# Attention units taken chunk by chunk through the batches, with two narrow first groups and stores by tile

## What is computed

```python
f = 1.0 / (1.0 + np.exp(-f_logit))
for t in range(S):
    state = f[:, :, t, :, None] * state + einsum('bhd,bhe->bhde', k[:, :, t], v[:, :, t])
    y[:, :, t] = einsum('bhd,bhde->bhe', q[:, :, t], state)
x = y as (B * S, H * D)                      # 3072 tokens of 384
h = x @ w_in                                 # 384 -> 2048
x = (maximum(h, 0) + log1p(exp(-abs(h)))) @ w_out
h = x @ moe2_w_in
x = where(h >= 1, h, where(h <= -1, 0, (h + 1)**2 / 4)) @ moe2_w_out
```

## Time and profile before

| | |
|---|---|
| median of three runs | 954.64 us (952.54 to 954.88) |
| profiled execution, its own time | 954.34 us |
| its span, first to last instruction | 952.6 us |
| TensorE matmuls busy | 909.5 us, 95% |
| VectorE, ScalarE, GpSimd busy | 538.1, 446.2 and 84.6 us |
| mean granted TensorE clock | 0.985 |
| bytes moved by DMA | 49.8 MB, mean 52 GB/s |

### The profile page before, as it was taken

One profiled execution on the slowest core, in us unless ns is written; L12 is line 12 of the kernel. 1 busy time (PEld: TensorE's weight loads), 2 busy tenths in 40 slices (PEclk: granted clock), 3 DMA queues, 4 the chain that ended last, 5 costly groups with the idle time before them and its releaser, 6 DMA issues.

```text
span 952.6 us, 14831 instructions
## 1 busy us (share of the span) xinstructions
PE 909.5 (95%) x5742; PEld 765.7 (80%) x5742; DVE 538.1 (56%) x925; ACT 446.2 (47%) x837; POOL 84.6 (9%) x66
## 2 busy tenths in 40 slices
PE   5569999899999999999999999999999999999996
PEld 3469999889778787877888888888888888888885
DVE  4965576665655656566435555455555554554543
ACT  3465666556554655565467743233323333332322
POOL 3321021211210111012000010000000000000000
PEclk8789999999999999999999999999999999999998
DMA  9631133223212132131012210020010200200001
GB/s 214 190 94 40 39 81 63 57 55 64 65 40 55 57 71 47 40 119 54 1 67 86 81 67 0 1 67 1 20 47 0 67 1 1 67 1 1 33 1 36
DMA packets 18811, 49.77 MB, mean 52 GB/s; under 512 B 1968, under 2 KB 3120, under 8 KB 18736
## 3 DMA queue, kind: packets, MB, share of 16 engines
q1 hardware_dynamic: 18736, 48.77, 19.5%
HBM read 39.32 MB, written 9.44 MB: 51 GB/s over the span
## 4 chain that ended last, share of the span: by engine, by line
PE 87%; DVE 6%; issue 3%; ACT 2%; DMA 2%; POOL 0%; SPq 0%; DVEq 0%; ACTq 0%; POOLq 0%
PE h_ps L464 13%; PE y_ps L464 13%; PE h_ps L466 13%; PE y_ps L466 13%; PE h_ps L465 13%; PE y_ps L465 13%; PE a_ps L521 2%; PE c_ps L534 2%; PE a_ps L554 2%; DVE dec L805 1%; DVE g_lo L786 1%; PE c_ps L541 1%; PE c_ps L547 1%; PE c_ps L511 1%; DMA w_raw<-w 1%
## 5 line engine op out<-in xcount | busy, mean ns | idle before, releaser
L786 DVE TENSOR_TENSOR g_lo<-gate,g_hi 128x512 fp32r<-128x512 f32 (+2 forms) x208 | 142.4, 685 | 337.8 <-ACT g_hi L648 337.8
L464 PE MATMUL h_ps<-x_hi,w_hi 128*128 128x512 f32 (+2 forms) x624 | 238.0, 381 | 8.9 <-DVE gate L770 7.2
L464 PE MATMUL y_ps<-g_hi,w_hi 128*128 128x512 f32 (+2 forms) x624 | 234.3, 376 | 9.0 <-DVE y_sb L792 4.7
L465 PE MATMUL h_ps<-x_lo,w_hi 128*128 128x512 f32 (+2 forms) x624 | 233.3, 374 | 0.0
L466 PE MATMUL h_ps<-x_hi,w_lo 128*128 128x512 f32 (+2 forms) x624 | 233.2, 374 | 0.0
L466 PE MATMUL y_ps<-g_hi,w_lo 128*128 128x512 f32 (+2 forms) x624 | 232.7, 373 | 0.0
L465 PE MATMUL y_ps<-g_lo,w_hi 128*128 128x512 f32 (+2 forms) x624 | 232.7, 373 | 0.0
L636 ACT ACTIVATE soft<-h_ps 128x512 f32<-128x512 f32 x96 | 57.4, 598 | 260.0 <-PE h_ps L466 260.0
L464 PEld LDWEIGHTS y_ps<-g_hi,w_hi 128*128 128x128 f32 x624 | 117.6, 188 | 32.5 <-DVE g_lo L786 13.7
L464 PEld LDWEIGHTS h_ps<-x_hi,w_hi 128*128 128x128 f32 x624 | 117.7, 189 | 31.6 <-DVE w_lo L867 7.7
L632 ACT ACTIVATE soft<-h_ps 128x512 f32<-128x512 f32 (+2 forms) x112 | 60.1, 536 | 166.5 <-PE h_ps L466 166.4
(11 more groups left out here) (76 smaller groups left out, 660.9 us busy)
## 6 DMA issues: line engine op xcount, KB each, us to landing
qkf_sb<-qkf SPq DMA_DIRECT2D x48, 288.0 KB, 5.0
w_raw<-w SPq DMA_DIRECT2D x32, 384.0 KB, 5.3
v_sb<-v SPq DMA_DIRECT2D x24, 320.0 KB, 5.3
qkf_sb<-x_mid SPq DMA_DIRECT2D x6, 768.0 KB, 6.2
out<-y_sb SPq DMA_DIRECT2D x6, 768.0 KB, 3.9
x_mid<-y_sb SPq DMA_DIRECT2D x4, 768.0 KB, 4.0
x_mid<-y_sb SPq DMA_DIRECT2D x2, 576.0 KB, 3.4
x_mid<-y_sb SPq DMA_DIRECT2D x1, 384.0 KB, 2.8
```

What stands on the lines that cost most here:

```text
L464: nc.tensor.matmul(out_ap, hi1, hi2, start=start, stop=False, skip_group_check=True)
L465: nc.tensor.matmul(out_ap, hi1, lo2, start=False, stop=False, skip_group_check=True)
L786: nc.vector.tensor_tensor(g_lo[:, t % 2, 0:g.n], gate[:, t % 2, 0:g.n], g_hi[:, t % 2, 0:g.n].bitcast(F32), ALU.subtract).then_inc(glo_don ...
```

## The change

- **Order of the units.** Unit u is now chunk u // 4 of batch u % 4. The state is kept for each batch; the first four units have no state to read and the last four leave none. The host lays the inputs out so, and turns the output back.
- **First groups.** Layer 0 has groups of 2, 2, 4, 4, 4, 4, 4 units instead of 3, 2, 3, 4, 4, 4, 4. The prologue does units 0 and 1 with their own buffers (scores and turned keys of unit 1 in y_sb), with keys and queries multiplied on VectorE and the plus one on ScalarE. Weight slices 0 to 2 get their low part from GpSimd, 3 from VectorE; slices 4 to 15 are split in group 0's slots (`first_splits`), four slots ahead of their use. The increments of units 0 and 1 stand behind `up(0)` and `up(1)`. Units 2 and 3 have their main stages spread over slots m to m + 4.
- **Loads.** The padding rows come from DRAM; the memsets are gone. A unit has three loads with semaphores of their own: f, qk and v (112 rows of 2 KB and of 4 KB, 128 rows of 2 KB).
- **State and v.** The state is 64 columns a pair, read by TensorE without stride: eight matmuls with 48 rows and four with 112. v has 64 columns a head. The increment is eight matmuls of 64 or 48 stationary columns by 64 instead of four of 112 by 96. VectorE updates the state with two operations of 112 rows instead of four of 48.
- **Slots.** MAIN for 4 units is (0, 4, 8, 12) instead of (2, 5, 9, 12). The last scan and the second Newton operation come behind g_lo in their slot (`prep_end`). `dec` has two buffers.
- **Tiles stored singly.** Each y_ps tile has its own semaphores, ScalarE copies tile 0 as soon as it is complete, and each tile is stored by its own DMA.

```diff
-SIZES = ((3, 2, 3, 4, 4, 4, 4), ...
-MAIN = {2: (4, 9), 3: (3, 7, 11), 4: (2, 5, 9, 12)}
+SIZES = ((2, 2, 4, 4, 4, 4, 4), ...
+MAIN = {2: (7, 12), 3: (3, 7, 11), 4: (0, 4, 8, 12)}
 PREP = (-5, -4, -3, -1)
-STAGES = 4
+STAGES = (0, 1, 2, 3)
+EARLY_STAGES = (0, 1, 3, 4)
+EARLY_STAGES_PE = (0, 2, 3, 4)
...
+        def first_splits(slot):
+            return range(slot + 4, min(slot + 5, FT)) if slot > 2 else range(EARLY, slot + 5)
...
+                load_f(0)
+                load_f(1)
+                load_qk(0)
+                load_qk(1)
+                load_v(0)
+                load_v(1)
+                for m in range(4):
+                    load_w(m)
+                load_unit(2)
+                for m in range(4, RAW):
+                    load_w(m)
+                for m in range(RAW, RAW + 3):
+                    load_w(m)
                 unit_left(0)
                 load_unit(3)
+                load_w(RAW + 3)
+                unit_left(1)
+                load_unit(4)
...
+                for k in range(KT):
+                    sp.wait_ge(y_ps_free[k], g.G + 2)
+                    sp.dma_start(to[:, k, g.token:g.token + g.n], y_sb[:, k, 0:g.n]).then_inc(y_sb_free, 16)
...
+            def increment(u):
+                a_ps, kt = banks(u)[0], k_tok_of(u)
+                for p in range(PAIRS):
+                    for a, cols in ((0, slice(0, 64)), (1, slice(64, ROWS))):
+                        h = 2 * p + a
+                        mm = nc.tensor.matmul(a_ps[cols, p * HEAD:(p + 1) * HEAD], kt[:, p, cols],
+                                              v_sb[:, u % RING, h * HEAD:(h + 1) * HEAD],
+                                              start=True, stop=True, skip_group_check=True)
...
+            pe.wait_ge(consts, 6)
             keep_warm(3)
-            first_group(prep, main, no_split)
-            keep_warm(1)
+            turn_keys(0)
+            keep_warm(2)
+            turn_keys(1)
+            keep_warm(3)
+            score(0)
+            score(1)
+            result(0)
+            result(1)
             up(LAYER0[0], 0)
             up(LAYER0[0], 1)
+            increment(0)
+            increment(1)
+            pe.wait_ge(state_done, FIRST)
...
             def copy_y(g):
-                act.wait_ge(y_done, FT * (g.G + 1))
-                act.wait_ge(y_sb_free, 16 * (g.G + 1))
-                for k in range(2):
-                    nc.scalar.activation(y_sb[:, k, 0:g.n], y_ps[k][:, 0:g.n], ACT.Copy).then_inc(y_ps_free, 1)
+                act.wait_ge(y_sb_free, 16 * KT * (g.G + 1))
+                for k in range(KT - 1):
+                    act.wait_ge(y_tile_done[k], g.G + 1)
+                    nc.scalar.activation(y_sb[:, k, 0:g.n], y_ps[k][:, 0:g.n], ACT.Copy).then_inc(y_ps_free[k], 1)
...
+            prep(0, 1)
+            prep_end(0, 1)
+            keys(0)
+            prep(1, 1)
+            prep_end(1, 1)
+            keys(1)
+            prep(0, 3)
+            prep_end(0, 3)
+            queries(0)
+            prep(1, 3)
+            prep_end(1, 3)
+            queries(1)
+            main(0, 1)
+            main(1, 1)
+            main(0, 3)
+            main(1, 3)
+            split_w(3)
             gated(LAYER0[0], 0)
+            main(0, 2)
             split_lo(LAYER0[0], 0)
-            rest_of_first(prep, split_w)
+            main(1, 2)
```

More of the change, by code:

```diff
@@ L102, in prep_at, with batch, has_past, has_future @@
         return []
[L103 to L111, removed]
+    return [(u, PREP.index(at - m)) for u, m in MAIN_SLOT.items() if at - m in PREP]
+def batch(u):
+    return u % B
+def has_past(u):
+    return u >= B
+def has_future(u):
+    return u < UNITS - B
+def states_until(u):
+    return min(u + 1, UNITS - B)
 def build(nc, qkf, v, w, out, x_mid):
@@ L539, in main @@
                         for j in range(4):
-                            h = 4 * tile + j
-                            nc.tensor.matmul(c_ps[HALF * j:HALF * (j + 1), t], v_sb[:, slot, h * D:h * D + HALF],
-                                             scores[:, h % 2, h // 2, :], start=False, stop=True, skip_group_check=True)
+                            pair, rows = 2 * tile + j // 2, slice(64 * (j % 2), 64 * (j % 2) + D)
+                            nc.tensor.matmul(c_ps[HALF * j:HALF * (j + 1), t], st[rows, pair, 0:HALF],
+                                             q[rows, pair, :], start=(tile == 0), stop=False, skip_group_check=True)
@@ new lines, in result @@
+                pe.wait_ge(v_in[u % RING], 16 * (u // RING + 1))
+                pe.wait_ge(masked, 2 * u + 2)
+                for tile in range(2):
+                    t = slice(tile * P, (tile + 1) * P)
+                    for j in range(4):
+                        h = 4 * tile + j
+                        nc.tensor.matmul(c_ps[HALF * j:HALF * (j + 1), t], v_sb[:, u % RING, h * HEAD:h * HEAD + HALF],
+                                         sc[:, h % 2, h // 2, :], start=(tile == 0 and not has_past(u)),
+                                         stop=True, skip_group_check=True)
@@ L564, in body, with main @@
+            def main(u, s):
+                if s == 0:
+                    turn_keys(u)
+                    score(u)
+                if s == 1:
+                    result(u)
+                    if has_future(u):
+                        increment(u)
             def body(g):
@@ L893, in body @@
                     gated(of, t)
+                    for m in first_splits(slot) if g.G == 0 else ():
+                        split_w(m)
                     for u, s in main_at(g, slot):
```

438 lines of the change are left out of this document (208 added, 230 removed).

## The result

The changed kernel takes 920.58 us (median of four runs, 918.61 to 925.53) against 953.72 for the kernel before on the same chip: a ratio of 0.966, 95% interval 0.962 to 0.970. The forecast was 936.5, with a range of 925 to 949. The sign is right, the gain of 33 us is nearly twice the 18 forecast, and the time lies outside the range.

A forecast was written before the change was run, and what follows sets the result against it. The prediction took TensorE to bound the kernel: its wait before the first feed-forward matmul, its work and its standing. Its terms summed to -18.0 us from 954.34, giving 936.3 in the profiled execution, stated as 936.5, range 925 to 949.

The forecast's parts named there:

- First `up`: Prologue: the first feed-forward matmul starts at about 21.5 us instead of 45.46, -24.0 us.
- One more unit, increments of units 0 and 1, no state for 2 and 3: TensorE work behind the first `up`: +4.0 us, +1.6 us and -1.4 us.
- New shapes: Increment and state blocks: smaller tiles, taken to overlap in pairs, cost +1.5 us, range -1 to +12.
- Group 0: First group's body: 15 us of TensorE standing instead of 9.5, three engines equally full, +5.5 us.
- feeds keep up: ScalarE and VectorE run ahead, group 0 loses 9 us, not 15, and boundary waits vanish: 929 us; chance 0.24.
- The two-unit group: Group 1: four units prepared beside 256-wide slots instead of three, +1.5 us.
- Wide groups: 4-wide boundaries and slots: 8.9 us of layer 0 waits fall to 3.5 us, -5 us, bounds -8 and +2.
- Tail: End of the run: the last tile, stored singly, is issued earlier and lands sooner, -1.7 us.
- Unpaired increments: Increment block: column tiles do not overlap in pairs, +8 us; 944.5 us, chance 0.23 shared with a starved group 0.
- Starved group 0: Group 0: weight slices 9 and up queue behind unit loads, +7 us; 944.5 us, chance 0.23 shared with unpaired increments.
- Half clock in the narrow groups: Two narrow groups: the granted clock stays at half, 965 us with 20 slow slots; chance 0.04.
- Late prologue: Prologue: unit loads hold the first matmul to 40 us or later, giving 955 us; chance 0.02.

The follow-up runs named there:

- f4: Changed kernel without the eight useless `keep_warm` matmuls in the prologue; 923.39 us.
- f3: Changed kernel with nine extra, unused ScalarE copies of 512 columns ahead of weight splits in group 0; 922.41 us.
- e3: Changed kernel with the last scan and second Newton operation ahead of the weight split (g_lo) on VectorE again; 921.36 us.
- f1: Changed kernel with slots 2, 5, 9, 12, last scan and second Newton step ahead of g_lo, whole copies and one store; 925.64 us.
- f5: Changed kernel with slots 2, 5, 9, 12 and each unit's preparation whole ahead of g_lo, unit by unit; 932.87 us.
- g1: Kernel before with `dec` twice and preparations split, second parts after all first parts, still ahead of g_lo; 945.59 us against 952.75.
- g2: Kernel before with only the main parts of 4-unit groups moved to slots 0, 4, 8, 12; 943.01 us, ratio 0.989.
- e4: Changed kernel with one store and one wait for the three y_ps tiles instead of single ones; 921.76 us.
- f2: Changed kernel with old slots, old order ahead of g_lo, one store, and the state update in four operations of 48 rows; 927.79 us.
- i1: Changed kernel with the wait for the first two states put behind `up(2)` and unit 3's main stage one slot earlier; 922.61 us.

## Why the prediction was wrong

**First `up`: -24.0 forecast, -25.5 measured.** The chain of the text gave 19.7, and 19.95 came; f landed at 3.9, the scans start at 5.32 as forecast, the qk load was late by 0.9 us. The failed step is the addition of 1.8 us for `keep_warm` and loads. f4 shows that the extra matmuls shorten the chain. That 19.7 fits within 0.3 us is in part luck, as the late load was not in it.

**One more unit, increments of units 0 and 1, no state for 2 and 3: +4.2 forecast.** By the counts of blocks in both traces this is +4.3.

**New shapes: +1.5 forecast, -1.4 measured** (20 increments, each 0.2 us less, and 20 state blocks, each 0.13 more). I took pairs to overlap but no gain from it, though the figure used, 16 instructions at 29 ns, already gave 0.46 against the 0.81 of the old block. The upper figure of +4 took the 0.1 us of one change for each of the drains that the Trainium skill ("TensorEngine Tiling (Array Packing)", Key Properties) tells of at a change of tiling mode. It fell: the state block with its 48-row tiles and its change of mode costs 0.13 us more in all. With +0.3 us for slots of 256 instead of 384 columns these terms give the +3.1 of the account within 0.1 us.

**Group 0: +5.5 forecast, -1.4 measured.** Before, it stood 11.2 us, not 9.5. After, it stood 9.8, not the 15 of the forecast, and here the failed step is "if each slot took what its longest engine takes the group would be 57". The rows of the windows view (length, busy time of PE, PEld, DVE, ACT, POOL, granted clock, DMA share, GB/s) for group 0 from slot 2 to slot 2, and for most of the two-unit group:

```profile
24.46:77.77 53.31, 47.43 (x516) 43.96 (x516) 43.88 (x85) 40.52 (x96) 9.00 (x7) 1.00 0.39 123
77.77:126.00 48.23, 47.83 (x569) 44.62 (x566) 36.00 (x79) 30.85 (x78) 9.07 (x7) 1.00 0.30 89
```

ScalarE has 40.5 us of work where I had put 45, VectorE 43.9 for 41, and the group takes 53.3, with 4.0 us for the two blocks of unit 4 in it that the 57 leaves out. The engines run ahead of each other between waits, so an uneven slot is made good by the next; f3 shows it directly, 5.4 us more work for 2.2 us more time, clock included. The order of the preparation has little share: undone alone it cost 2.2 us in this group, 1.5 of them by the clock (e3), undone with the slots nothing (f1, f5). The rival "feeds keep up" named this and gave 929, for which it lacked the next points.

**The two-unit group: +1.5 forecast, -0.6 measured.** The step took four units beside narrow slots to overfill ScalarE and VectorE. It holds for the old order and slots: in f5 this group takes 62.2 us, nearly half of the excess by the clock, in the changed kernel 54.2. The forecast gave the new order no credit here.

**Wide groups: -5 forecast, -10.3 measured.** The step that failed is the cause given for the earlier trace rows and the 3.5 us of waits that it left standing: "a copy of y_sb stands behind preparation on VectorE". That is so, but the preparation was 1 us longer than its work, and I had priced slots by the usual duration of their instructions. All 8.9 us of the eight gaps went. Had I listed the durations of the scans along the run, eight of them at 2.35 would have stood out. g1, g2 and f5 show this cause: standing in the wide groups changes by -6.9, -10.1 and +5.1 us, the whole times by -7.2, -9.7 and +12.3. The meeting itself is 0.98 us of VectorE a time, 8 us in sum; what stays open is how the rest divides. g2 takes away the slow scans and also spreads other work, and f5 still stands less in the wide groups than the kernel before (11.0 against 16.2 us, in groups that are not the same). No run has f5's edits and the single store together.

**Tail: -1.7 forecast, +0.5 measured.** The median landing did fall, to 2.2 us on the page. But in this execution the last store took 5.2 us to land, 1.4 of them its issue: three issues in a row take 3.07 us on the queue, which the forecast, with one issue at 0.38, left out. By all profiles (see e4) the term is about -1, and the +0.5 belongs to this pair of executions.

**Rivals.** Unpaired increments: refuted by 0.61 us. Starved group 0: refuted by its 9.8 us. Half clock in the narrow groups: refuted, granted clock 1.00 in both windows above; but spells of 3.4 or 6.8 us at 0.50 came there in e3, f2, f3, f4, f5 and i1, so its mechanism exists, only far shorter than the rival had it. Late prologue: refuted by 19.95.

## What to carry to other kernels

List the duration of one instruction along the run, not only its mean: where the same shape takes 1.37 us in one slot and 2.35 in another, see which other engine runs beside it. An order that keeps VectorE's two-input work away from GpSimd's products where a slot has no time left can be worth 1% without an instruction less, and it shows in an undo experiment only when everything that keeps them apart is undone together. Before a term of 1 or 2 us is judged by one pair of profiles, look at the same term in the others. A sum of each slot's longest engine overstates the time of a group whose engines may run ahead.

## What the runs showed of the hardware

- Four scans on VectorE of 1.37 us take 2.35 beside a GpSimd product, g_lo 1.24 instead of 0.69, and the plus one 0.92 to 1.41 instead of 0.42; where the scan started first GpSimd took 1.99 instead of 1.41.
- Three stores issued one behind the other held the queue for 3.07 us, one alone for 0.38; the last of three took 0.43 to 1.56 in eight profiles.
- 64- and 48-column increments overlap as pairs: 16 instructions in 0.49 us.
- Without the `keep_warm` matmuls TensorE ran the prologue's result blocks in 1.08 instead of 0.65 us.
- A wait of 2.2 us before `up(16)` was followed by a granted clock of 0.50 for 3.4 us in f4 and by 1.00 in the changed kernel; a spell of 3.4 us cost some 1.4 us.
